# The last product of each expert group over 128 rows instead of 64, and at least one block per expert

## The chip, the cores and the metric

The kernel runs on one core of a Trainium2 chip. The metric is the time of one execution on the device in microseconds (us); lower is better.

## The reference, cut to what matters

Three stages follow each other. The first is a recurrent attention over 768 steps for 4 x 8 heads of 40. Its output, 3072 tokens of 320 numbers, goes through two mixtures of 8 experts with a hidden size of 1024:

```
# stage one: every token goes to one expert, at most 384 tokens each
logits = x @ w_gate
for idx in argsort(-logits.flatten()):          # best pairs first
    tok, e = idx // E, idx % E
    if assigned[tok] < 0 and counts[e] < cap:
        assigned[tok] = e; counts[e] += 1
out[mask] = maximum(x[mask] @ w1[e], 0) @ w2[e]

# stage two: every token goes to its best expert, without a limit
logits = (x / |x|) @ (emb / |emb|).T / tau
expert_idx = argmax(logits); gate_w = softmax(logits)[expert_idx]
for e in range(E):
    mask = expert_idx == e
    if not mask.any(): continue
    out[mask] = gate_w[mask] * (maximum(x[mask] @ w1[e], 0) @ w2[e])
```

The tokens of an expert in stage two are as many as fall to it: 324, 391, 241, 410, 350, 615, 235 and 506 for the inputs that the reference draws.

## The kernel before

Every engine has its own program, and semaphores order them. The attention takes the first 205 us or so, the routing of stage one goes on to about 450 us. The prediction is about the two expert stages behind it.

Float32 products are made of parts: a number is its high part (type fp32r) and a low part, what the rounding to the high part leaves. A product of w and x is w_hi x_hi + w_hi x_lo + w_lo x_hi, three matmuls. The 320 numbers of a token are three slices of the contraction, of 128, 128 and 64. For the third slice, w1_hi holds the high part of w1 in its rows 0 to 63 and the low part in rows 64 to 127, and xT_hi holds the same 64 numbers twice, so that one matmul over 128 rows (L1331, L1424) makes w_hi x_hi + w_lo x_hi. What is left is w_hi x_lo of the third slice, a matmul over the 64 rows 0 to LOW - 1 (L1332, L1425). It is the last of the eight that fill a PSUM bank, and carries the semaphore.

**Stage one** (step3, eight steps, one per expert, 384 tokens each). up3 goes through the eight 128-column parts f of the hidden layer: eight matmuls of 384 columns into bank f % 2. ACT takes the bank with a relu into hT_hi (L446), DVE makes hT_lo from bank and hT_hi (L959) and so frees the bank; PE waits for that before it fills the bank again, two parts later (hl3_done). Then turn3 transposes the tokens of the next expert (L1316), ACT and DVE make xT_hi and xT_lo of it (L439, L953), and down3 multiplies the hidden layer with w2 for three blocks of 128 tokens (L1304 to L1306). Between them lie the routing of stage two for the results of the step before: transposes (L1251), logits (L1361) and ranks (L1370).

**Stage two** (experts2, 31 blocks of 128 tokens, whose expert is read from a table). A step is: up(i), for two halves of the hidden layer, eight matmuls of 512 columns each; turn(i + 1), three transposes (L1407); down(i - 1); turn_hidden(i), eight transposes (L1443). ACT makes hid (L499), xT_hi (L503) and hT_hi (L514), DVE xT_lo (L1060), hT_lo (L1067) and the weighted result (L1072).

**The table** of stage two's blocks is computed by DVE after the last routing (L1108 to L1134): nblk is the number of blocks of each expert, cumb their running sum, and from it come the expert, the place of the weights and the first row of each block. row_ready (L1126) releases ACT's loads of token rows, tab_ready (L1134) the other engines. Of the 31 blocks those behind the last expert's are filling.

**The weights** of both stages pass through two places (RING). SP loads the raw w1 and w2 of an expert into one buffer each; it asks for w1 when POOL is done with the last w1, for w2 when POOL is done with the last w2. POOL copies raw weights by DMA into the high parts (L625, L627 for w1, L646 for w2), then subtracts to get the low parts (L634, L636, L652). In stage two SP also hands PE's progress on to POOL, behind its own loads in its queue:

```
done = sp.value_load(cumb_i[0:1, m:m + 1], min_val=0, max_val=NB2)
sp.wait_ge(h_ready, 2 * done + 1)
sp.sem_inc(slot1_free, 1)
sp.wait_ge(yb_ready, done + 1 + G)
sp.sem_inc(slot2_free, 1)
```

When POOL is done with the weights of the last expert, it scatters the results of stage two to the output, block by block (L682).

Of the kernel before, what the change touches and what calls it, by code (L numbers as in the profile page):

```python
# [45 lines left out]
KT = 3  # L46
# [20 lines left out]
class Chain:  # L67
# [14 lines left out]
    def link(self, ins):  # L82
        self.need(self.mark(ins))


def build(nc, t, out):
    ctx = ExitStack()
    with ctx:
# [598 lines left out]
        def _(dve):  # L687
# [261 lines left out]
            def x_lo3(e, p):  # L949

                for k in range(KT):
                    dve.wait_ge(xh3_ready, KT * e + k + 1)
                    V.tensor_tensor(xT_lo[:, k, :], bank[2 + k][:, 0:BPE * 128], xT_hi[:, k, :], ALU.subtract).then_inc(xl3_done, 1)  # L953
                V.tensor_copy(ids3[:, p, :], rows[:, :, XROW - 2]).then_inc(ids3_ready, 1)  # L954

            def hidden_lo3(e):
# [100 lines left out]
            def x_lo(i, s):  # L1057

                dve.wait_ge(xh_ready, i + 1)
                V.tensor_tensor(xT_lo[:, :, 0:128], bank[2][:, 0:384].rearrange("p (k t) -> p k t", k=KT), xT_hi[:, :, 0:128], ALU.subtract)  # L1060
                V.tensor_copy(ids[:, ds(i, 1)], rows[:, s, XROW - 2:XROW - 1])
                V.tensor_copy(weight[:, ds(i, 1)], rows[:, s, XROW - 1:XROW]).then_inc(x_done, 1)

# [28 lines left out]

            link(V.tensor_tensor(emb_sq[:, :], emb[:, :], emb[:, :], ALU.mult))
            V.tensor_reduce(emb_n[:, 0:1], emb_sq[:, :], AX.X, ALU.add).then_inc(sqrt_in, 1)
            V.memset(prev3[:, :, :], 0.0)
            V.tensor_copy(offset[:, :], region[:, :])
            link(V.reciprocal(tau[:, :], tau[:, :]))
# [12 lines left out]

            link(V.tensor_tensor(work[:, :, :], by_expert(rem[:, :]), g128[:, :, :], ALU.is_gt))
            link(V.tensor_reduce(nblk[:, :], work[:, :, :], AX.X, ALU.add))
            link(V.memset(full[:, :], 1.0))
            link(V.tensor_tensor_scan(cumb[:, :], full[:, :], nblk[:, :], 0.0, ALU.mult, ALU.add))

# [23 lines left out]
        def _(pe):  # L1139
# [179 lines left out]
            def up3(e, s):  # L1319

                pe.wait_ge(w1_ready, 2 * e + 2)
                pe.wait_ge(xl3_done, KT * (e + 2))
                for f in range(FT):
                    dst, cols = bank[f % 2][:, 0:BPE * 128], slice(f * 128, (f + 1) * 128)
                    pe.wait_ge(hl3_done, FT * e + f + 1)
                    for k in range(2):
                        T.matmul(dst, w1_hi[:, s, k, cols], xT_hi[:, k, :], start=(k == 0), stop=False)  # L1327
                        T.matmul(dst, w1_hi[:, s, k, cols], xT_lo[:, k, :], start=False, stop=False)  # L1328
                        T.matmul(dst, w1_lo[:, s, k, cols], xT_hi[:, k, :], start=False, stop=False)  # L1329

                    T.matmul(dst, w1_hi[:, s, 2, cols], xT_hi[:, 2, :], start=False, stop=False)  # L1331
                    T.matmul(dst, w1_hi[0:LOW, s, 2, cols], xT_lo[0:LOW, 2, :], start=False, stop=True).then_inc(h3_ready, 1)  # L1332

            def down3(e, s, b):
                dst, cols = bank[5 + b][:, 0:DM], slice(b * 128, (b + 1) * 128)
# [74 lines left out]
            def up(i):  # L1410
# [8 lines left out]
                for f in range(2):  # L1419
                    for k in range(2):  # L1420
                        products(bank[f][:, :], xT_hi[:, k, 0:128], xT_lo[:, k, 0:128],
                                 w1_part(w1_hi, 128, k, f), w1_part(w1_lo, 128, k, f), k == 0, False)

                    T.matmul(bank[f][:, :], xT_hi[:, 2, 0:128], w1_part(w1_hi, 128, 2, f), start=False, stop=False)  # L1424
                    T.matmul(bank[f][:, :], xT_lo[0:LOW, 2, 0:128], w1_part(w1_hi, LOW, 2, f), start=False, stop=True).then_inc(h_ready, 1)  # L1425

            def down(i):
                slot = pe.value_load(tab2[0:1, 0, ds(i, 1)], min_val=0, max_val=RING - 1)
# [106 lines left out]
```

## Time and profile before

| | us |
|---|---|
| median of 3 runs | 1084.75 |
| lowest, highest | 1078.61, 1091.55 |
| span of the profiled execution | 1103.3 |
| time of the profiled execution | not given beside its span |
| PE busy | 816.0 (74%) |
| DVE busy | 567.8 (51%) |
| POOL busy | 392.8 (36%) |
| ACT busy | 217.4 (20%) |

The span goes from the first to the last instruction of the execution that the profiler recorded; it is longer than any of the three runs. Busy shares are means over stages with different limits. PE stands for TensorE's matmuls and PEld for its weight loads, which have a row of their own; the ends of matmuls are modelled by the profiler, their starts are measured. A time that stands ahead of "<-" is idle time of the engine just before the instruction, and the name behind it is what ended it; "issue" means that nothing in the profile did.

### The profile page before, as it was taken

How to read it: one execution, taken by the hardware profiler on the slowest of the kernel's cores; microseconds unless marked ns; L12 is line 12 of the kernel's file. 1: busy time of each engine (PE TensorE's matmuls, PEld its weight loads, DVE VectorE, ACT ScalarE, POOL GpSimd, SP SyncE). 2: the span in 40 equal slices, each digit the busy share in tenths (PEclk: the TensorE clock that was granted, in tenths of full speed). 3: DMA queues.
4: the chain of work that ended last, by engine and by line, in shares of the span. 5: the costliest groups of instructions: out<-in, count | busy, mean ns of one | idle time of the engine just before them, and what ended most of it. 6: DMA issues, size and time to landing. Idle time of an engine off the chain costs nothing.

```text
span 1103.3 us, 18868 instructions
## 1 busy us (share of the span) xinstructions
PE 816.0 (74%) x5803; PEld 679.3 (62%) x5804; DVE 567.8 (51%) x1558; ACT 217.4 (20%) x451; POOL 392.8 (36%) x334
## 2 busy tenths in 40 slices
PE   2989888982233333039999999994799999998496
PEld 1777777861222222028888888874577888776385
DVE  7877778357766677302656566648222222222121
ACT  3221222000000000002332322331222222221121
POOL 4443334035200000533554465546034254356411
PEclk9998899695555555559999888996899999999699
DMA  4444443264300000233766576555454755653200
GB/s 133 136 142 119 130 119 107 68 196 127 122 0 0 0 0 0 78 109 83 247 193 189 185 236 197 150 175 172 132 174 125 215 171 167 191 156 118 89 27 1
DMA packets 70227, 137.26 MB, mean 124 GB/s; under 512 B 14791, under 2 KB 53968, under 8 KB 66098
## 3 DMA queue, kind: packets, MB, share of 16 engines
q1 hardware_dynamic: 43282, 67.16, 20.8%
q0 software_dynamic: 11008, 58.16, 16.2%
q10 hardware_dynamic: 15904, 11.53, 4.0%
q8 instruction: 17, 0.28, 0.1%
q14 instruction: 16, 0.13, 0.0%
HBM read 77.36 MB, written 14.48 MB: 83 GB/s over the span
## 4 chain that ended last, share of the span: by engine, by line
PE 53%; DVE 17%; issue 9%; another core or an unknown queue 1%; ACT 1%; DVEq 0%; POOL 0%; ACTq 0%; POOLq 0%
PE bank L1304 8%; PE bank L1305 7%; PE bank L1306 7%; PE bank L1290 4%; PE bank L1327 3%; PE bank L1425 2%; PE bank L1443 2%; PE bank L1332 2%; PE bank L1328 2%; PE bank L1329 2%; PE bank L1259 2%; PE bank L1361 2%; DVE routing_arena L859 2%; DVE routing_arena L892 2%; DVE routing_arena L954 1%
## 5 line engine op out<-in xcount | busy, mean ns | idle before, releaser
L1304 PE MATMUL bank<-w_hi,hT_hi 128*128 (+1 forms) x440 | 148.3, 337 | 19.1 <-issue 16.5
L1306 PE MATMUL bank<-w_hi,hT_lo 128*128 (+1 forms) x440 | 142.7, 324 | 1.8 <-issue 1.8
L1305 PE MATMUL bank<-w_lo,hT_hi 128*128 (+1 forms) x440 | 143.3, 326 | 1.0 <-issue 1.0
L1290 PE MATMUL bank<-routing_arena 128*8 128x16 bf16 x1344 | 43.3, 173 | 103.7 <-DVE routing_arena L859 103.7
L652 POOL TENSOR_TENSOR w_lo<-w_raw,w_hi 128x2560 fp32r<-128x2560 f32 x16 | 91.0, 5685 | 76.1 <-DMA w_hi<-w_raw 75.6
L606 POOL DMA_INDIRECT x_sorted<-tokens,routing_arena x48 | 47.3, 986 | 187.7 <-DVE routing_arena L942 161.6
L1290 PEld LDWEIGHTS bank<-routing_arena 128*8 128x8 bf16 x1344 | 37.5, 93 | 108.8 <-DVE routing_arena L859 108.8
L1304 PEld LDWEIGHTS bank<-w_hi,hT_hi 128*128 128x128 f32 x440 | 89.5, 203 | 21.9 <-issue 21.7
L634 POOL TENSOR_TENSOR w_lo<-w_raw,w_hi 128x2048 fp32r<-128x2048 f32 x16 | 73.0, 4564 | 69.0 <-DMA w_hi<-w_raw 68.1
L1305 PEld LDWEIGHTS bank<-w_lo,hT_hi 128*128 128x128 f32 x440 | 89.5, 203 | 1.8 <-issue 1.8
L1306 PEld LDWEIGHTS bank<-w_hi,hT_lo 128*128 128x128 f32 x440 | 89.1, 202 | 1.4 <-issue 1.4
L1060 DVE TENSOR_TENSOR xT_lo<-bank,xT_hi 128x384 fp32r<-128x384 f32 x31 | 17.3, 557 | 135.5 <-ACT xT_hi L503 135.5
L959 DVE SCALAR_TENSOR_TENSOR hT_lo<-bank,hT_hi 128x384 fp32r<-128x384 f32 x64 | 35.7, 557 | 80.2 <-ACT hT_hi L446 79.0
L625 POOL DMA_DIRECT2D w_hi<-w_raw x16 | 9.3, 582 | 160.5 <-PE bank L1332 79.7
L1202 PE MATMUL bank<-mlstm_arena 128*128 128x41 f32 (+3 forms) x384 | 62.1, 291 | 0.0
L1178 PE MATMUL bank<-mlstm_arena 128*128 128x256 f32 x192 | 55.6, 432 | 7.8 <-DVE mlstm_arena L736 7.8
L1304 PE MATMUL bank<-w_hi,xT_hi 128*128 x124 | 55.5, 447 | 7.4 <-issue 4.6
L1072 DVE TENSOR_SCALAR tokens<-bank,routing_arena 128x320 f32 (+1 forms) x31 | 17.1, 551 | 83.2 <-PE bank L1306 75.4
L725 DVE TENSOR_TENSOR_SCAN mlstm_arena<-bank,mlstm_arena 128x384 f32<-128x384 f32 x64 | 57.3, 940 | 3.7 <-PE bank L1167 3.2
L499 ACT ACTIVATE routing_arena<-bank 128x512 f32<-128x512 f32 x62 | 37.0, 600 | 112.3 <-PE bank L1425 94.7
L1202 PEld LDWEIGHTS bank<-mlstm_arena 128*128 128x128 f32 x384 | 57.8, 214 | 1.2 <-issue 0.2
L514 ACT ACTIVATE hT_hi<-bank 128x512 fp32r<-128x512 f32 x62 | 33.9, 596 | 118.7 <-PE bank L1443 98.8
(250 smaller groups left out, 1806.7 us busy)
## 6 DMA issues: line engine op xcount, KB each, us to landing
w_raw<-in_moe_w SPq DMA_DIRECT2D x16, 1280.0 KB, 6.7
w_hi<-w_raw POOLq DMA_DIRECT2D x16, 1280.0 KB
w_raw<-in_moe_w SPq DMA_DIRECT2D x16, 1024.0 KB
w_hi<-w_raw POOLq DMA_DIRECT2D x16, 1024.0 KB, 4.7
w_hi<-w_raw POOLq DMA_DIRECT2D x32, 256.0 KB, 5.8
mlstm_arena<-in_q SPq DMA_DIRECT2D x64, 120.0 KB
routing_arena<-x_sorted ACTq DMA_DIRECT2D x31, 160.0 KB
w_raw<-in_moe_w SPq DMA_DIRECT2D x16, 256.0 KB
```

Source lines behind the costliest of these rows:

```text
L499: nc.scalar.activation(hid[:, f * 512:(f + 1) * 512], bank[f][:, :], ACT.Relu).then_inc(relu_done, 1)
L606: pool.indirect_dma_start(dst, bass.IndirectOffsetOnAxis(ap=dest[:, g:g + 1], axis=0), tokens[:, slot, :], None).then_inc(scattered, 16)
L634: nc.gpsimd.tensor_tensor(w1_lo[:, s, :, :], w1_raw[:, 0:2, :], w1_hi[:, s, 0:2, :], ALU.subtract).then_inc(w1_ready, 1)
L652: nc.gpsimd.tensor_tensor(w2_lo[:, s, :, :], w2_raw[:, :, :], w2_hi[:, s, :, :], ALU.subtract).then_inc(w2_ready, 1)
L725: V.tensor_tensor_scan(decay[:, h, c], bank[f][:, 0:HALF], diag[:, :], 0.0, ALU.mult, ALU.add).then_inc(decay_done, 1)
L959: V.scalar_tensor_tensor(hT_lo[:, f, :], bank[f % 2][:, 0:BPE * 128], 0.0, hT_hi[:, f, :], ALU.max, ALU.subtract).then_inc(hl3_done, 1)
L1178: last = T.matmul(bank[2 + (NQ * k + g) % 2][:, c * QC:(c + 1) * QC], kT[:, s, chunk * CH:(chunk + 1) * CH], q_apart[:, s, chunk, :, :].re ...
L1202: last = T.matmul(bank[6 + s][:, at:at + n], probs[:, 2 * s + h, c * CH:(c + 1) * CH], v_in[:, 2 * s + h, c * DV:c * DV + n], start=(c == ...
L1290: last = T.matmul(bank[6][0:E, 0:WAYS], choice[:, :, g], cmp_b[:, g, :], start=(g == 0), stop=(g == G - 1))
L1304: T.matmul(dst, a_hi, b_hi, start=first, stop=False)
L1305: T.matmul(dst, a_hi, b_lo, start=False, stop=False)
L1306: return T.matmul(dst, a_lo, b_hi, start=False, stop=last)
```

## The change

- The matmuls L1332 and L1425, w1_hi by xT_lo of the third slice, take all 128 rows. Rows 64 to 127 of w1_hi hold w1's low part there.
- Rows 64 to 127 of xT_lo's third slice are cleared once (a memset of DVE ahead of stage one), so that they add nothing, and the instructions that write xT_lo leave them alone: in stage one the one for the third slice is cut to 64 partitions, in stage two one instruction for three slices becomes two (128 partitions by two slices, 64 by one).
- In the table of stage two the number of blocks of an expert is at least 1: one DVE instruction more.

```diff
@@ x_lo3 (DVE, stage one)
-                    V.tensor_tensor(xT_lo[:, k, :], bank[2 + k][:, 0:BPE * 128], xT_hi[:, k, :], ALU.subtract).then_inc(xl3_done, 1)
+                    V.tensor_tensor(xT_lo[0:KP[k], k, :], bank[2 + k][0:KP[k], 0:BPE * 128], xT_hi[0:KP[k], k, :], ALU.subtract).then_inc(xl3_done, 1)
@@ x_lo (DVE, stage two)
-                V.tensor_tensor(xT_lo[:, :, 0:128], bank[2][:, 0:384].rearrange("p (k t) -> p k t", k=KT), xT_hi[:, :, 0:128], ALU.subtract)
+                V.tensor_tensor(xT_lo[:, 0:2, 0:128], bank[2][:, 0:256].rearrange("p (k t) -> p k t", k=2), xT_hi[:, 0:2, 0:128], ALU.subtract)
+                V.tensor_tensor(xT_lo[0:LOW, 2, 0:128], bank[2][0:LOW, 256:384], xT_hi[0:LOW, 2, 0:128], ALU.subtract)
@@ DVE, ahead of stage one
+            V.memset(xT_lo[LOW:128, 2, :].bitcast(fp32), 0.0)
@@ DVE, table of stage two
             link(V.tensor_reduce(nblk[:, :], work[:, :, :], AX.X, ALU.add))
+            link(V.tensor_scalar(nblk[:, :], nblk[:, :], 1.0, None, ALU.max))
@@ up3 (PE, stage one)
-                    T.matmul(dst, w1_hi[0:LOW, s, 2, cols], xT_lo[0:LOW, 2, :], start=False, stop=True).then_inc(h3_ready, 1)
+                    T.matmul(dst, w1_hi[:, s, 2, cols], xT_lo[:, 2, :], start=False, stop=True).then_inc(h3_ready, 1)
@@ up (PE, stage two)
-                    T.matmul(bank[f][:, :], xT_lo[0:LOW, 2, 0:128], w1_part(w1_hi, LOW, 2, f), start=False, stop=True).then_inc(h_ready, 1)
+                    T.matmul(bank[f][:, :], xT_lo[:, 2, 0:128], w1_part(w1_hi, 128, 2, f), start=False, stop=True).then_inc(h_ready, 1)
```

## Rows read from the trace of the kernel before

**Rows 1.** The page, part 4: the chain that ended last, shares by engine.
```profile
PE 53%; DVE 17%; issue 9%; another core or an unknown queue 1%; ACT 1%; DVEq 0%; POOL 0%; ACTq 0%; POOLq 0%
```

**Rows 2.** Windows of 20 us: window, length, busy by engine, clock, DMA, GB/s.
```profile
core 0: us, PE busy (x) PEld busy (x) DVE busy (x) ACT busy (x) POOL busy (x), PEclk, DMA share, GB/s
...
640.00:660.00 20.00, 19.33 (x96) 17.08 (x96) 11.28 (x39) 6.65 (x14) 11.14 (x7) 0.83 0.80 251
...
880.00:900.00 20.00, 20.00 (x115) 16.53 (x114) 6.20 (x14) 6.43 (x12) 8.73 (x4) 1.00 0.52 156
...
1020.00:1040.00 20.00, 4.74 (x17) 4.20 (x18) 1.39 (x2) 1.45 (x3) 12.43 (x13) 0.59 0.31 111
```

**Rows 3.** Timeline of stage one, one group of eight products: start, length, engine, line.
```profile
655.33 0.44 PE L1332 MATMUL bank<-xT_lo,w_hi 64*128 64x384 f32 x1
...
655.80 0.49 ACT L446 ACTIVATE hT_hi<-bank 128x384 fp32r<-128x384 f32 x1 [1.23 <-PE bank L1332]
655.98 0.34 PE L1328 MATMUL bank<-xT_lo,w_hi 128*128 128x384 f32 x1
...
656.33 0.56 DVE L959 SCALAR_TENSOR_TENSOR hT_lo<-bank,hT_hi 128x384 fp32r<-128x384 f32 x1 [1.17 <-ACT hT_hi L446]
...
656.84 0.34 PE L1331 MATMUL bank<-xT_hi,w_hi 128*128 128x384 f32 x1
657.11 0.44 PE L1332 MATMUL bank<-xT_lo,w_hi 64*128 64x384 f32 x1
```

**Rows 4.** Timeline of stage two, across the end of a half in up.
```profile
986.22 0.39 PE L1424 MATMUL bank<-w_hi,xT_hi 128*128 x1
...
986.53 0.18 PEld L1425 LDWEIGHTS bank<-w_hi,xT_lo 64*128 64x128 f32 x1 [0.35 <-issue]
...
986.97 0.50 PE L1304 MATMUL bank<-w_hi,xT_hi 128*128 x1
...
987.30 0.39 PE L1305 MATMUL bank<-w_lo,xT_hi 128*128 x1
...
987.52 0.39 PE L1306 MATMUL bank<-w_hi,xT_lo 128*128 x1
```

**Rows 5.** Groups of weight loads by form, both stages: busy, mean ns, idle before.
```profile
L1332 PEld LDWEIGHTS bank<-xT_lo,w_hi 64*128 64x128 f32 x64 | 11.8, 184 | 16.2 <-issue 16.2
...
L1425 PEld LDWEIGHTS bank<-w_hi,xT_lo 64*128 64x128 f32 x62 | 11.3, 183 | 22.5 <-issue 22.5
```

**Rows 6.** Timeline of POOL in stage two: weights of experts 3, 4 and 7.
```profile
838.54 0.57 POOL L625 DMA_DIRECT2D w_hi<-w_raw  x1 [6.77 <-SPq L391]
...
845.42 4.59 POOL L634 TENSOR_TENSOR w_lo<-w_raw,w_hi 128x2048 fp32r<-128x2048 f32 x1 [5.28 <-DMA w_hi<-w_raw]
...
871.78 0.57 POOL L625 DMA_DIRECT2D w_hi<-w_raw  x1 [2.06 <-SPq L391]
...
882.09 4.59 POOL L634 TENSOR_TENSOR w_lo<-w_raw,w_hi 128x2048 fp32r<-128x2048 f32 x1 [8.71 <-DMA w_hi<-w_raw]
...
990.89 2.42 POOL L636 TENSOR_TENSOR w_hi<-w_raw,w_hi 64x1024 fp32r<-64x1024 f32 x1
```

**Rows 7.** Timeline of PE and ACT, 993 to 1042 us: block 23 and the hole.
```profile
993.87 0.47 PE L1304 MATMUL bank<-w_hi,xT_hi 128*128 x1
...
1002.24 1.03 PE L1443 MATMUL bank<-ident,routing_arena 128*128 128x128 f32 x8
...
1011.39 1.03 PE L1443 MATMUL bank<-ident,routing_arena 128*128 128x128 f32 x8
...
1022.77 0.60 ACT L514 ACTIVATE hT_hi<-bank 128x512 fp32r<-128x512 f32 x1 [14.19 <-remote]
...
1041.94 1.91 PE L1443 MATMUL bank<-ident,routing_arena 128*128 128x128 f32 x8
```

**Rows 8.** The page, part 5: DVE's subtraction of the tokens in stage two.
```profile
L1060 DVE TENSOR_TENSOR xT_lo<-bank,xT_hi 128x384 fp32r<-128x384 f32 x31 | 17.3, 557 | 135.5 <-ACT xT_hi L503 135.5
```

**Rows 9.** Timeline of DVE in the table of stage two.
```profile
766.57 0.16 DVE L1127 TENSOR_SCALAR routing_arena<-routing_arena 128x31 f32<-128x31 f32 x1
...
766.76 5.47 DVE L1128 TENSOR_SCALAR routing_arena<-routing_arena 128x31 f32<-128x31 f32 x1
```

## The prediction

> **What bounds the kernel now.** I read the chain that ended last first: over half of it is TensorE, with VectorE far behind [rows 1]. The windows then say where: in both expert stages (about 487 to 761 us and 775 us to the end) PE is busy for the whole of a window such as 880 to 900 us, at the full 2.4 GHz, while DVE, ACT and POOL are idle most of it [rows 2]. So there PE's own instructions set the time, and the question is how densely they follow each other. Two things interrupt this: in stage one part of each step runs at 1.2 GHz (window 640 to 660 has 0.83 of full speed, and 2 x 0.17 x 20 makes 6.8 us at half) [rows 2], and near the end, in window 1020 to 1040, there is a hole [rows 2], to which I return.
>
> Then the timeline of one group of eight products in stage one [rows 3]. Products with 128 rows start 0.172 us apart (655.98 to 656.84 is five of them). The product with 64 rows (L1332) starts 0.27 us after its forerunner (656.84 to 657.11), and from one L1332 to the next it is 1.78 us, where eight products at 0.172 make 1.38. In stage two [rows 4] the full products are 0.22 to 0.23 apart. The weight load of the 64-row product starts at 986.53, 0.31 after the matmul before it started and 0.08 before that one's end. The next matmul starts 0.43 after L1425's load, and the one behind it 0.33 later. A weight load of the same shape as its neighbour starts with the matmul ahead of it, so it is hidden; at each change of the row count it isn't. The grouped rows show that this is regular: 64 and 62 such loads, each preceded by an idle loader, 16.2 and 22.5 us in all, while a load itself takes the usual 0.18 us [rows 5].
>
> **Part one, 128 rows instead of 64, stage one (L1332, 64 times).** If the full-row product behaves like its seven neighbours, a group takes 1.38 instead of 1.78: 0.40 saved. What is late next is the eviction. From the start of L1332 it is 0.47 to ACT's start, 0.53 more to DVE's, and 0.56 for DVE [rows 3]; a full-row matmul ends about 0.1 earlier, so 1.46, and I estimate 0.04 to 0.1 for the way back to PE (ACT and DVE start 0.03 to 0.04 after the end of what they wait for). The bank is wanted again one product and one group after the start of L1332: 0.17 + 1.38 = 1.55. The two are equal within my reading. If PE has to wait, it also pays an unhidden load, 0.10 by the last step of [rows 4], every second group or every group, and the gain is near 0.32. I take 0.36, the middle. The last of the eight groups of a step leads into the down product, which waits for that same eviction in series, so I count 0.15 there. A step gains 7 x 0.36 + 0.15 = 2.7, eight steps 21 us (18 to 25).
>
> **Part one, stage two (L1425, 62 times).** For the first half of the hidden columns, 986.22 to 987.30 is 1.08 where three pitches of 0.23 are 0.69: 0.39. The second half is followed by small transposes, which hide the last 0.10: 0.29. A block gains 0.68, and 31 blocks would give 21 us. I don't count all of it, since weights are supplied by POOL at a pace of its own. POOL's copy for expert 3 began at 838.54, released by the SP line that passes on PE's progress; for expert 4 at 871.78, where it had only just finished the work before (idle 2.06) [rows 6]. From there the supply is a closed loop (SP issues the next raw load when POOL is done, POOL waits for DMA), and PE's progress doesn't enter. The third slice of the last expert's w1 was ready at 990.89 + 2.42 = 993.31, and PE's block 23, the first of that expert, started at 993.87 [rows 6, 7]: a margin of 0.6 us. With 0.68 less per block PE would be there 23 x 0.68 = 15.6 us earlier, and finds no weights.
>
> How far does the supply itself come forward? Its last release by PE is the one at 838.54, after the seventh block: 7 x 0.68 = 4.8 us earlier. But then POOL's copy meets the raw load of w2 that SP has just issued. For expert 3 the wait for this copy was 5.28, for expert 4, where it met that load, 8.71 [rows 6], a difference of 3.4; moving into part of that load costs an estimated 1.8 of the 4.8. So the supply moves by 3 us (1.4 to 4.8) and block 23 with it. After it 7 blocks of 0.68 are PE's own: 4.8. Stage two gains 3 + 4.8 = 7.8. PE's new waits, 15.6 - 3 = 12.6 us shared by the later experts, may let the clock fall, as it does in the hole below (window 1020 to 1040 at 0.59) [rows 2]; I give 0 to 3 us for this and take 0, since what a slower clock costs ahead of the next wait is taken off that wait.
>
> **The hole.** From PE's turn of the hidden rows at 1002.24 to the next at 1011.39 is 9.15; to the one after it 30.55, so 21.4 us are lost [rows 7]. ACT stood still for 14.19, by a release that the profile can't name, although its input was there; POOL meanwhile issues its saved-up output scatters back to back (13 POOL instructions in window 1020 to 1040) [rows 2]. They start when POOL's last weights are done, wherever PE is, and both move by about 3 us here, so I keep the loss as it is, with 8 us either way.
>
> **Part two, the rest.** The subtraction of stage two (L1060, 557 ns, 31 times) becomes two instructions; one more costs DVE at most another 0.56 per block, during the down product, and DVE waited 135.5 us in all before it, more than 4 per block [rows 8]: nothing. Should that cover go, it is 0.56 per block. The clearing of xT_lo's lower rows runs once while all engines wait for the scatters before stage one: nothing. In stage one the subtraction only has fewer partitions. The bound of at least one block per expert adds one small DVE instruction ahead of the block table, about 0.2 us, the distance from L1127 to L1128. There DVE is about to be held: L1128, 31 elements a row like L1127, took 5.47 us in place of 0.16 [rows 9]. One instruction more means that a different one is held, with up to two left for later: 0 to 0.6 us; I take 0.2. It changes no block count if every expert has tokens, and the release of POOL at 838.54 just after seven blocks fits the counts of the reference's own inputs (3, 7, 9, 13, 16, 21, 23, 27 blocks cumulated), where the least is two.
>
> **A rule against this change.** What the rows show is that a 64-row load lasts 0.18 us like the full ones [rows 5], and only the waiting differs. The Trainium skill (TensorE: Matmul & The Clock Gate, Part 2, on LDWEIGHTS) says that the row count doesn't matter for the load's time; taken alone that gives a gain of nothing. The Trainium skill (TensorEngine Tiling (Array Packing), Key Properties) says "Changing tiling mode (not just tile) drains the TensorE", which is what the two gaps look like; by it the whole of both gaps goes. Rows here have the gaps but not their cause.
>
> **The sum.** 21 + 7.8 - 0.2 = 28.6, say 29 us. The profiled execution spans 1103.3 us and would span 1074; no other time of it is given. It lies 18.6 above the median of the runs, 1084.75, part of which may be the hole. Carried over as it is: 1084.75 - 29 = 1056.
>
> **Rivals.** (a) The weights don't hold stage two (POOL's loop shortens too): 21 + 21, stage one at up to 25: 1039 to 1043. Against it: POOL's waits are DMA times. 10%. (b) The gaps aren't due to the rows but to the last product of a group (its semaphore, its operand), so the change doesn't do what it says: 1085. For it: every 64-row product is also the last of its accumulation, so the rows can't separate them. Against: the loader is idle ahead of the 64-row load too [rows 5], and no semaphore stands between L1424 and L1425 in the code. 8%. The rule of the Trainium skill (TensorE: Matmul & The Clock Gate, Part 2) that the row count doesn't matter ends here too. (c) Slower: the clock. Stage one spends some 6.8 us of a step at 1.2 GHz [rows 2]; each us there costs 0.5. If the new waits (on evictions in stage one, on weights in stage two) keep PE at 1.2 GHz for 58 us more, the 29 are used up, at 100 more it is 1084.75 + 21 = 1106. Against: in stage one the waits are hundredths of a us, and full-row products raise the load. 3%. (d) The forecast's mechanism with the hole grown or shrunk: inside the range.
>
> **Chances.** Forecast 79%, (a) 10%, (b) 8%, (c) 3%. The range: low end (a), 1039. High end: stage one 18, stage two 5, the hole 8 longer, gives 1070, and 4 for a median of three runs that spread over 13: 1074. One per cent, 10.8 us, is about what a measurement of this kernel can tell from nothing. Faster by over 1%: 0.87 (forecast nearly whole, (a)); within: 0.10; slower: 0.03.
>
> **What the profile after would show.** The idle time ahead of the loads of L1332 and L1425 gone, groups of 1.38 to 1.46 us in stage one, the step shorter by 2.5 to 3 us; blocks of 8.5 us in stage two, and new PE waits of 4 us or so ahead of an expert's first block, above all block 23, released by POOL's L636; the table's DVE instructions held as before; the hole in the same place. I'd be wrong if the gap stays ahead of the last product, if PE doesn't wait before block 23, or if the hole changes by over 8 us.

## The result, and the profile after

| | before | changed |
|---|---|---|
| median, us | 1081.68 (4 runs) | 1053.20 (4 runs) |
| lowest, highest | 1078.25, 1091.55 | 1047.95, 1055.98 |
| span of the profiled execution | 1103.3 | 1051.0 |
| its time | - | 1052.89 |

The ratio is 0.9718, with a 95% interval of 0.9669 to 0.9767: 28.5 us between the medians and 30.5 between the means, from which the ratio is taken (25 to 36 by its interval), where 29 were forecast. The median of before was 1084.75 over three runs in the prediction; with the fourth it is 1081.68, so the forecast of 1056 lies 2.8 above the measured 1053.20. The time is 1.9 above the span (1052.89 and 1051.0).

The page of the changed kernel, part 1 and the shares of the chain that ended last (part 4), which answer to [rows 1]:

```profile
PE 768.7 (73%) x5803; PEld 683.1 (65%) x5804; DVE 572.6 (54%) x1591; ACT 216.4 (21%) x451; POOL 392.9 (37%) x334
...
PE 38%; DVE 18%; issue 10%; DMA 8%; POOL 6%; ACT 1%; SPq 0%; DVEq 0%; ACTq 0%; POOLq 0%
```

PE's share of the chain fell from 53% to 38%, and DMA and POOL now hold 14%: from block 23 the chain goes back through the supply of weights. PE lost 47 us of busy time (816.0 to 768.7), since the gaps had counted as busy. Against a second profile of before, which has no hole (e1, below), it is 43.5 us (812.2 to 768.7) for a span that is 30.0 shorter (1081.0 to 1051.0): some 13.5 us of what the full-row products saved came back as idle time of PE, 4 in stage one and 10 in stage two.

**Stage one.** The changed kernel's timeline of PE, PEld, ACT and DVE, where L1330 to L1334 are the seven full products and L1335 is the last one, now over 128 rows. It answers to [rows 3]:

```profile
643.36 0.34 PE L1335 MATMUL bank<-xT_lo,w_hi 128*128 128x384 f32 x1
...
644.27 0.56 DVE L959 SCALAR_TENSOR_TENSOR hT_lo<-bank,hT_hi 128x384 fp32r<-128x384 f32 x1 [0.95 <-ACT hT_hi L446]
...
644.61 0.33 PE L1334 MATMUL bank<-xT_hi,w_hi 128*128 128x384 f32 x1
...
644.78 0.34 PE L1335 MATMUL bank<-xT_lo,w_hi 128*128 128x384 f32 x1
644.88 0.19 PEld L1330 LDWEIGHTS bank<-xT_hi,w_hi 128*128 128x128 f32 x1
644.96 0.36 PE L1330 MATMUL bank<-xT_hi,w_hi 128*128 128x384 f32 x1
```

L1335 follows its forerunner by 0.17 (644.61 to 644.78) where it was 0.27, and a group takes 1.42 (643.36 to 644.78) where it took 1.78. The load at 644.88 doesn't start with L1335, as loads do elsewhere in the group, but 0.10 later and 0.05 after the end of DVE's eviction (644.27 + 0.56): that is the new limit. The groups by form, which answer to [rows 5], show no idle time before the last product in stage one and 2.6 us in all in stage two, where there were 22.5:

```profile
L1335 PEld LDWEIGHTS bank<-xT_lo,w_hi 128*128 128x128 f32 x64 | 12.2, 191 | 0.0
...
L1428 PEld LDWEIGHTS bank<-w_hi,xT_lo 128*128 128x128 f32 x62 | 11.9, 192 | 2.6
```

From the first transpose of stage one to the first of stage two (the eight steps and the table) it is 269.49 us (483.69 to 753.18). Before it was 288.44 in the profile that the prediction used, 285.71 in a second one (below). That is 16 to 19 us.

**Stage two.** The timeline of PE across the end of the first half, which answers to [rows 4]:

```profile
889.92 0.39 PE L1427 MATMUL bank<-w_hi,xT_hi 128*128 x1
890.15 0.39 PE L1428 MATMUL bank<-w_hi,xT_lo 128*128 x1
890.38 0.39 PE L1307 MATMUL bank<-w_hi,xT_hi 128*128 x1
```

All are 0.23 apart. A block without a wait takes 8.38 instead of 9.16, so 0.78 less where 0.68 was forecast. From 753.18 to the end it is 297.82 us; before it was 327.99, or 305.7 without the hole (21.4, and 0.9 in the block behind it, whose turn of the hidden rows comes after 10.04 instead of 9.15), and 307.85 in the second profile. That is 8 to 10 us of the 24 that 31 blocks of 0.78 would make. Where the rest went is seen at POOL and PE, whose timelines answer to [rows 6, 7]:

```profile
813.23 0.57 POOL L625 DMA_DIRECT2D w_hi<-w_raw  x1 [6.38 <-SPq L391]
...
964.59 2.34 POOL L636 TENSOR_TENSOR w_hi<-w_raw,w_hi 64x1024 fp32r<-64x1024 f32 x1
```

```profile
967.17 0.79 PE L1307 MATMUL bank<-w_hi,xT_hi 128*128 x1 [3.28 <-POOL w_hi L636]
967.76 0.63 PE L1308 MATMUL bank<-w_lo,xT_hi 128*128 x1
...
973.21 0.39 PE L1427 MATMUL bank<-w_hi,xT_hi 128*128 x1
```

PE waits for the weights of the last expert (block 23) by name, 3.28 us. Then its products last 0.63 instead of 0.39 for 6 us: 1.2 GHz (the granted clock of the window 967 to 973 is 0.50). One other wait for weights is named, 2.25 us for L652 at 913.01, behind the first block of the sixth expert. Besides waits for DVE of 4.6 us, which were there before, the rest of PE's idle time in stage two has no name in the trace: "issue" ahead of blocks, up to 1.45 us at once, 8 us in all, where the second profile of before has 4. Counted from stage two's start, the release for expert 3 is at 60.05 (before 63.23), the end of the last third slice at 213.75 (before 218.0), and block 23 at 213.99 (before 218.56).

**The hole** is not there. POOL's burst of scatters runs from 979.02, and the blocks beside it take 8.37.

### The profile page after: what moved, and what is told of

The parts are those of the page before. It is cut to its first block, busy times and chain, and to the rows that moved or that the text cites. A ratio compares the mean times of both kernels' runs of the same rounds, so it can differ in the third digit from the quotient of the medians.

```text
span 1051.0 us, 18901 instructions
## 1 busy us (share of the span) xinstructions
PE 768.7 (73%) x5803; PEld 683.1 (65%) x5804; DVE 572.6 (54%) x1591; ACT 216.4 (21%) x451; POOL 392.9 (37%) x334
## 3 DMA queue, kind: packets, MB, share of 16 engines
q1 hardware_dynamic: 43282, 67.16, 21.4%
## 4 chain that ended last, share of the span: by engine, by line
PE 38%; DVE 18%; issue 10%; DMA 8%; POOL 6%; ACT 1%; SPq 0%; DVEq 0%; ACTq 0%; POOLq 0%
DMA w_hi<-w_raw 8%; PE bank L1307 5%; PE bank L1308 4%; PE bank L1309 4%; PE bank L1293 4%; PE bank L1330 2%; PE bank L1262 2%; POOL w_lo L634 2%; PE bank L1331 2%; PE bank L1332 2%; POOL w_lo L652 2%; PE bank L1364 2%; DVE routing_arena L859 2%; DVE routing_arena L892 2%; DVE routing_arena L954 2%
## 5 line engine op out<-in xcount | busy, mean ns | idle before, releaser
L1308 PE MATMUL bank<-w_lo,hT_hi 128*128 (+1 forms) x440 | 141.0, 320 | 0.0
L652 POOL TENSOR_TENSOR w_lo<-w_raw,w_hi 128x2560 fp32r<-128x2560 f32 x16 | 91.1, 5692 | 72.9 <-DMA w_hi<-w_raw 72.4
L634 POOL TENSOR_TENSOR w_lo<-w_raw,w_hi 128x2048 fp32r<-128x2048 f32 x16 | 73.0, 4564 | 72.3 <-DMA w_hi<-w_raw 71.5
L1060 DVE TENSOR_TENSOR xT_lo<-bank,xT_hi 128x256 fp32r<-128x256 f32 x31 | 13.2, 425 | 119.0 <-ACT xT_hi L503 119.0
L959 DVE SCALAR_TENSOR_TENSOR hT_lo<-bank,hT_hi 128x384 fp32r<-128x384 f32 x64 | 35.7, 558 | 58.3 <-ACT hT_hi L446 58.3
L1307 PE MATMUL bank<-w_hi,xT_hi 128*128 x124 | 53.3, 430 | 13.1 <-issue 7.0
L1205 PE MATMUL bank<-mlstm_arena 128*128 128x41 f32 (+3 forms) x384 | 59.8, 283 | 0.2 <-ACT mlstm_arena L429 0.2
L1205 PEld LDWEIGHTS bank<-mlstm_arena 128*128 128x128 f32 x384 | 55.4, 205 | 1.6 <-issue 0.5
```

What stands on the lines that cost most here:

```text
L634: nc.gpsimd.tensor_tensor(w1_lo[:, s, :, :], w1_raw[:, 0:2, :], w1_hi[:, s, 0:2, :], ALU.subtract).then_inc(w1_ready, 1)
L652: nc.gpsimd.tensor_tensor(w2_lo[:, s, :, :], w2_raw[:, :, :], w2_hi[:, s, :, :], ALU.subtract).then_inc(w2_ready, 1)
L959: V.scalar_tensor_tensor(hT_lo[:, f, :], bank[f % 2][:, 0:BPE * 128], 0.0, hT_hi[:, f, :], ALU.max, ALU.subtract).then_inc(hl3_done, 1)
L1205: last = T.matmul(bank[6 + s][:, at:at + n], probs[:, 2 * s + h, c * CH:(c + 1) * CH], v_in[:, 2 * s + h, c * DV:c * DV + n], start=(c == ...
L1307: T.matmul(dst, a_hi, b_hi, start=first, stop=False)
L1308: T.matmul(dst, a_hi, b_lo, start=False, stop=False)
```

## The experiments

Ratios are to the kernel before in runs on the same chip in the same job. Medians of before were 1082.61 (e1 to e4), 1082.76 (e5 to e8) and 1106.85 (e9 to e12); in the third job every kernel profiled had the hole, so absolute times are compared within a job only.

**e1_before_again.** The kernel before, unchanged, with a profile.

> The kernel before, profiled once more. My theory takes the hole near the end (21.4 us between two turns of the hidden rows while POOL issues its saved-up scatters, and all engines stand) for an accident of the one profiled execution, since the profile of the changed kernel has the same burst of scatters and no hole: here it is absent or of another size, the span is 1076 to 1090 us, and stage two takes some 306 us instead of 328. Rival, that the hole belongs to the kernel before and the change removed it: it is there again with 20 us or more, and the span is about 1103.

Time 1082.86, span 1081.0, stage two 307.85. The timeline of PE across block 23 and later:

```profile
1000.55 1.03 PE L1443 MATMUL bank<-ident,routing_arena 128*128 128x128 f32 x8
...
1009.70 1.04 PE L1443 MATMUL bank<-ident,routing_arena 128*128 128x128 f32 x8
...
1018.92 1.03 PE L1443 MATMUL bank<-ident,routing_arena 128*128 128x128 f32 x8
```

The turns are 9.15 and 9.22 apart, where [rows 7] have 30.55. The hole belonged to that execution, not to the kernel, and it made up the distance to the median: the profiled time would be 1103.3 + 1.9, 20.5 above 1084.75, for a hole of 21.4 (22.3 with the slower block behind it).

**e2_stage1_only** and **e3_stage2_only.** Before, with part one in one stage alone (the clearing and the cut subtraction come with either).

```diff
  e2: up3
-  T.matmul(dst, w1_hi[0:LOW, s, 2, cols], xT_lo[0:LOW, 2, :], start=False, stop=True).then_inc(h3_ready, 1)
+  T.matmul(dst, w1_hi[:, s, 2, cols], xT_lo[:, 2, :], start=False, stop=True).then_inc(h3_ready, 1)
  e3: up
-  T.matmul(bank[f][:, :], xT_lo[0:LOW, 2, 0:128], w1_part(w1_hi, LOW, 2, f), start=False, stop=True).then_inc(h_ready, 1)
+  T.matmul(bank[f][:, :], xT_lo[:, 2, 0:128], w1_part(w1_hi, 128, 2, f), start=False, stop=True).then_inc(h_ready, 1)
```

> Part one in stage one alone; stage two keeps its 64-row products. Theory (each change of the row count costs 0.2 us of TensorE's time, twice a group): 19 to 21 us less than before, ratio 0.981, groups of 1.42 us instead of 1.79, stage two as before. Rival, that the last product of a group waits for another reason: in this kernel also gone, so it doesn't tell those apart; rival that the gain came from stage two or from chance: ratio over 0.99.

> Part one in stage two alone. Theory: blocks of 8.38 instead of 9.16 us where PE is free, but PE then waits for POOL's weights, so that of 31 x 0.78 = 24 us only 8 to 10 come out: ratio 0.991 to 0.993. Rival (the supply doesn't bind): 22 to 24 us, ratio 0.979.

e2: 0.9855 (0.9824 to 0.9887), stage one 268.34, stage two 307.73, unchanged. e3: 0.9929 (0.9896 to 0.9962), stage one 286.02, stage two 297.72. So the parts have their gains where they are made, 15.7 and 7.7 us, and one doesn't feed the other; their sum of 23.4 is below the 30.5 that the ratio of the whole change makes, and agrees with it just within the intervals (3.4, 3.6 and 5.3 us). e2 stays below its forecast; the step that lacks is told below.

**e4_rows64_middle.** The rival that the gap belongs to the last product and not to its rows: the 64-row product is moved into the middle of the group, and a 128-row product is last and carries the semaphore. (The same in up.)

```diff
                         T.matmul(dst, w1_lo[:, s, k, cols], xT_hi[:, k, :], start=False, stop=False)
+                        if k == 0:
+                            T.matmul(dst, w1_hi[0:LOW, s, 2, cols], xT_lo[0:LOW, 2, :], start=False, stop=False)
-                    T.matmul(dst, w1_hi[:, s, 2, cols], xT_hi[:, 2, :], start=False, stop=False)
-                    T.matmul(dst, w1_hi[0:LOW, s, 2, cols], xT_lo[0:LOW, 2, :], start=False, stop=True).then_inc(h3_ready, 1)
+                    T.matmul(dst, w1_hi[:, s, 2, cols], xT_hi[:, 2, :], start=False, stop=True).then_inc(h3_ready, 1)
```

> The kernel before with the 64-row product moved from the last place of each group of eight to the fourth, in both stages; the last is now the 128-row product of the third slice. Theory (the cost lies at the change of the row count): the two gaps move with it, group 1.78 us, block 9.16 us, ratio 0.997 to 1.003. Rival (it is the last product with its semaphore that waits): no gap ahead of the fourth product, one stays at the end or none at all; if none, the ratio is near 0.972.

1.0034 (0.9995 to 1.0072). Timeline of PE and PEld, stage one; L1331 is the 64-row product, L1333 the last:

```profile
654.94 0.34 PE L1329 MATMUL bank<-xT_hi,w_lo 128*128 128x384 f32 x1
655.21 0.18 PEld L1331 LDWEIGHTS bank<-xT_lo,w_hi 64*128 64x128 f32 x1 [0.25 <-issue]
655.21 0.44 PE L1331 MATMUL bank<-xT_lo,w_hi 64*128 64x384 f32 x1
...
655.58 0.19 PEld L1327 LDWEIGHTS bank<-xT_hi,w_hi 128*128 128x128 f32 x1 [0.19 <-issue]
...
656.21 0.33 PE L1333 MATMUL bank<-xT_hi,w_hi 128*128 128x384 f32 x1
...
656.38 0.33 PE L1327 MATMUL bank<-xT_hi,w_hi 128*128 128x384 f32 x1
```

The idle time of the loader went with the 64-row product, on both of its sides (0.25 and 0.19), while the last product of the group is followed at 0.17. A block of stage two without a wait takes 9.20 to 9.21 (before 9.15 to 9.16). Rival (b) is refuted.

**e5_rows64_pairs.** If the cost lies in the change of the row count, two 64-row products side by side should pay it once: the product is last in every even group and first in every odd one.

```diff
+                    if f % 2:
+                        T.matmul(dst, w1_hi[0:LOW, s, 2, cols], xT_lo[0:LOW, 2, :], start=True, stop=False)
...
-                    T.matmul(dst, w1_hi[0:LOW, s, 2, cols], xT_lo[0:LOW, 2, :], start=False, stop=True).then_inc(h3_ready, 1)
+                    if f % 2 == 0:
+                        last = T.matmul(dst, w1_hi[0:LOW, s, 2, cols], xT_lo[0:LOW, 2, :], start=False, stop=True)
+                    last.then_inc(h3_ready, 1)
```

> The kernel before with the 64-row product last in even groups and first in odd ones, so that two of them stand side by side: two changes of the row count per two groups instead of four, with as many 64-row products. Theory (the cost is the change): two groups take 2 x 1.38 + 0.40 = 3.16 us or a little more for the eviction, where 2 x 1.79 stood; stage one gains about half of the 19, stage two blocks of 8.77, held by the weights in part; 13 to 17 us, ratio 0.984 to 0.988. Rival (each 64-row product costs 0.4 wherever it stands): ratio 1.000.

0.9908 (0.9874 to 0.9943). Timeline of PE and PEld, the two side by side (L1335, L1327) and the next pair:

```profile
656.45 0.34 PE L1333 MATMUL bank<-xT_hi,w_hi 128*128 128x384 f32 x1
...
656.72 0.44 PE L1335 MATMUL bank<-xT_lo,w_hi 64*128 64x384 f32 x1
656.82 0.19 PEld L1327 LDWEIGHTS bank<-xT_lo,w_hi 64*128 64x128 f32 x1
657.00 0.34 PE L1327 MATMUL bank<-xT_lo,w_hi 64*128 64x384 f32 x1
...
657.26 0.19 PEld L1329 LDWEIGHTS bank<-xT_hi,w_hi 128*128 128x128 f32 x1 [0.25 <-issue]
...
659.91 0.44 PE L1335 MATMUL bank<-xT_lo,w_hi 64*128 64x384 f32 x1
```

Two groups take 3.19 (656.72 to 659.91), where they took 2 x 1.78: one of the two costs of 0.40 is gone. The second 64-row load has no idle time before it. A block takes 8.80, halfway to 8.38. The total gained 10 us (0.9908 of 1082.76), less than the 13 to 17 expected: in stage one the third step took 35.43, of which more below, and stage two was held by the weights (the interval of block 23 is 15.8). The Trainium skill (TensorEngine Tiling (Array Packing), Key Properties) has it that a change of the tiling mode drains TensorE; e4 and e5 agree, at 0.40 us for a change of the row count and the change back; what TensorE does in that time no run shows.

**e6_short_lows.** Is it the supply of the weights that holds stage two? For the experts of stage two that POOL fills during the stage, the subtractions for w1_lo and w2_lo cover 64 of 1024 and 16 of 320 columns; the other low parts stay those of an earlier expert. This leaves out part of the computation.

```diff
-  nc.gpsimd.tensor_tensor(w1_lo[:, s, :, :], w1_raw[:, 0:2, :], w1_hi[:, s, 0:2, :], ALU.subtract).then_inc(w1_ready, 1)
+  nf = F if n < E + RING else 64
+  nc.gpsimd.tensor_tensor(w1_lo[:, s, :, 0:nf], w1_raw[:, 0:2, 0:nf], w1_hi[:, s, 0:2, 0:nf], ALU.subtract).then_inc(w1_ready, 1)
```

> The changed kernel, where POOL computes only 64 of the 1024 columns of w1's low part and 16 of the 320 of w2's for experts 2 to 7 of stage two; the rest of the low parts is that of older weights. Theory (PE waits for POOL's weights in stage two): POOL's loop shortens by some 9 us an expert, PE's waits ahead of experts and the slow clock behind the longest go, 12 to 16 us less than the changed kernel, ratio 0.957 to 0.961. Rival (the waits have another source, such as fetching instructions or the loads themselves): the waits stay, ratio 0.97.

0.9637 (0.9571 to 0.9703); stage two 288.37, 9.4 less than with the change alone, and no PE wait on POOL is left. So by the profiles weights held some 9 of the missing 14 to 16 us. The 12 to 16 expected were not reached, and in time the kernel is only 0.8% below the change alone (0.9718), with intervals that overlap. What remains are seven idle times of PE of 0.9 to 1.8 us that the trace gives to nothing; e1 has four of 0.8 to 1.0, so they aren't new.

**e7_early_copies.** The whole computation, with the supply loop changed: SP passes PE's progress on before it asks for the next raw load, and POOL issues w1's copy ahead of the subtraction for w2, so that the copy runs beside it.

The part on POOL (SP's lines are only moved):

```diff
-                split_weights(n)
+                load_hi1(n)
+                if n > E + RING:
+                    make_lo2(n - 1)
+                make_lo1(n)
+                load_hi2(n)
+            make_lo2(2 * E - 1)
```

> The changed kernel with the full computation; SP passes PE's progress on ahead of the raw load of w2, and POOL issues the copy of an expert's w1 before it subtracts for the last expert's w2, and the copy of w2 without waiting for its landing, as in stage one. Theory: the DMA waits of POOL (some 20 us of a loop of 34) lie beside its subtractions, PE doesn't wait in stage two: 12 to 16 us less than the changed kernel, ratio 0.957 to 0.961. Rival (the DMA queues are the bound, so the copies land no earlier when more of them overlap): under 4 us, ratio 0.968 to 0.972.

0.9687 (0.9613 to 0.976); stage two 290.78, 7.0 less than with the change alone. POOL's timeline shows the loop turned round:

```profile
871.72 0.55 POOL L624 DMA_DIRECT2D w_hi<-w_raw  x1 [12.57 <-SPq L367]
...
873.35 5.68 POOL L651 TENSOR_TENSOR w_lo<-w_raw,w_hi 128x2560 fp32r<-128x2560 f32 x1
879.18 4.62 POOL L633 TENSOR_TENSOR w_lo<-w_raw,w_hi 128x2048 fp32r<-128x2048 f32 x1
```

POOL waits 12.57 for PE's progress instead of 8 to 10 for a DMA: the copy is hidden behind L651. No PE wait on POOL is left here either, with the whole computation, so e6's gain doesn't hang on the work that it leaves out. In the profile this is the best stage two of the full computation, though 7.0 is half of the 12 to 16 expected; in time it can't be told from the change alone (0.9718).

**e8_short_eviction.** Why 1.42 and not 1.38 in stage one: DVE's eviction (L959) writes 128 of 384 columns. The low part of the hidden layer is left out for the rest.

```diff
-  V.scalar_tensor_tensor(hT_lo[:, f, :], bank[f % 2][:, 0:BPE * 128], 0.0, hT_hi[:, f, :],
+  V.scalar_tensor_tensor(hT_lo[:, f, 0:128], bank[f % 2][:, 0:128], 0.0, hT_hi[:, f, 0:128],
```

> The changed kernel, where in stage one DVE computes hT_lo for 128 of the 384 tokens of each group (the rest is zero), so that the eviction of a group is some 0.27 us shorter. Theory (a group takes 1.42 us instead of 1.38 because PE waits for the eviction every second group): groups of 1.38, and the down product starts 0.27 sooner: 2.2 + 2 = 4 us, ratio 0.968. Rival (1.42 is what the products take): groups of 1.42 and 2 us for the down product alone.

0.9723 (0.9656 to 0.9791). The last products start at 645.41, 646.79 and 648.18, 1.38 apart, so the 0.04 was the eviction, as the prediction had it. Its value was not found: of 4 us expected the last steps gave 0.3 each (30.8 instead of 31.1), and stage one as a whole took 269.21, since its third step had grown to 35.49. A step loses more elsewhere, as e11 shows.

**e9_pe_four_blocks** and **e10_all_four_blocks.** The idle times of PE that e6 and e7 left could belong to the loop in PE's program (two blocks a turn). e9 is e7 with four blocks a turn on PE, e10 with ACT and DVE as well.

```diff
-                with pe.Fori(0, NB2 // 2 - 1) as j:
-                    step(2 * j + 1, lambda: turn(2 * j + 2, 0, j + 2))
-                    step(2 * j + 2, lambda: turn(2 * j + 3, 1, j + 2))
+                with pe.Fori(0, (NB2 // 2 - 1) // 2) as j:
+                    step(4 * j + 1, lambda: turn(4 * j + 2, 0, 2 * j + 2))
...
+                    step(4 * j + 4, lambda: turn(4 * j + 5, 1, 2 * j + 3))
```

> The kernel of e7 (earlier copies), with TensorE's loop over the blocks of stage two unrolled to four blocks a turn, seven turns in place of fourteen; the instructions of a block are the same. Theory: with the weights there, what is left between the blocks (idle 0.3 to 1.8 us that no semaphore ends, mostly ahead of an up at the loop's end, only while weights are copied) is the fetching of instructions behind the jump; with half the jumps half of it goes, 3 to 5 us less than e7, ratio 0.964 to 0.966. Rival (it comes with the transfers, wherever the loop ends): as e7, 0.9687.

> As e9, with the loops of ACT and DVE over the blocks unrolled to four as well. Theory: their jumps are off the path, so this is as e9 within 2 us. Rival (their fetching delays the blocks too): 2 us or more below e9.

e9: 0.9674 (0.9611 to 0.9738), e10: 0.9645 (0.958 to 0.971), e7 had 0.9687: no difference that can be told, though the intervals of 7 us either way leave room for the 3 to 5 us expected. The trace decides more: PE's timeline in e9, with half the jumps, still has the idle times:

```profile
880.13 0.49 PE L1311 MATMUL bank<-w_hi,xT_hi 128*128 x1 [1.37 <-issue]
```

Their cause stays open. Both profiles contain the hole (block intervals of 21.8 and 18.1 in e9), so it also comes in kernels with the change.

**e11_short_lows_stage1.** Where do stage one's steps lose time? The theory is that POOL's subtractions hold DVE. The cut of e6, but for the weights that are made during stage one (RING up to E + RING) in place of those of stage two; again part of the computation is left out.

```diff
+                nf = F if not RING <= n < E + RING else 64
...
+                nd = DM if not RING <= n < E + RING else 16
```

> The changed kernel, where POOL computes only 64 of 1024 columns of w1's low part and 16 of 320 of w2's for the weights that it prepares during stage one (those of experts 2 to 7 of stage one and the first two of stage two); the rest is older. Theory: small DVE instructions on SBUF are held while POOL subtracts (5.3 to 5.6 us for 128 x 3), and in the step whose third-to-last place this takes the path PE waits 3 us for the logits; with short subtractions no DVE instruction is held over 1 us, the step of 34.6 us falls to 31 and each other step loses its 0.7 to 0.9 us wait ahead of L1364: 6 to 10 us less than the changed kernel, ratio 0.963 to 0.967. Rival (the hold costs nothing but that one step): 3 us, ratio 0.969. Rival (the step is longer for its transfers): no change, 0.972.

0.951 (0.9447 to 0.9572): more than any theory said. Stage one takes 242.82 instead of 269.49, its later steps 27.2 instead of 31.1. The changed kernel first, timeline of POOL, DVE and PE in its fourth step:

```profile
561.06 5.70 POOL L652 TENSOR_TENSOR w_lo<-w_raw,w_hi 128x2560 fp32r<-128x2560 f32 x1
561.20 5.58 DVE L954 COPY routing_arena<-routing_arena 128x3 f32<-128x3 f32 x1
566.71 0.15 DVE L965 COPY tokens<-routing_arena 128x3 f32<-128x3 f32 x1
...
567.07 4.53 POOL L634 TENSOR_TENSOR w_lo<-w_raw,w_hi 128x2048 fp32r<-128x2048 f32 x1 [0.31 <-DMA w_hi<-w_raw]
567.17 0.40 DVE L984 COPY routing_arena<-bank 128x256 f32<-128x256 f32 x1
...
568.96 2.29 PE L1364 MATMUL bank<-gate_weights,routing_arena 128*128 128x8 f32 x13 [0.67 <-DVE routing_arena L985]
```

A copy of three elements a row begins 0.14 after POOL's subtraction, ends with it and takes 5.58; its like takes 0.15. DVE's copies for the logits come late by that, and PE waits 0.67. Then the windows of 2 us (length, busy by engine, clock, DMA, GB/s), the changed kernel:

```profile
568.00:570.00 2.00, 1.33 (x11) 1.03 (x9) 1.23 (x5) 1.92 (x7) 2.00 (x1) 1.00 0.88 206
570.00:572.00 2.00, 2.00 (x11) 1.93 (x11) 0.64 (x3) 1.97 (x3) 1.92 (x2) 0.58 1.05 387
572.00:574.00 2.00, 2.00 (x8) 1.98 (x9) 2.00 (x1) 0.56 (x1) 2.00 (x1) 0.50 1.04 331
574.00:576.00 2.00, 2.00 (x10) 2.00 (x9) 1.69 (x10) 0.00 (x0) 0.04 (x1) 0.50 0.40 62
576.00:578.00 2.00, 2.00 (x12) 2.00 (x11) 0.72 (x6) 0.22 (x1) 0.00 (x0) 0.72 1.03 422
```

and e11 at the same place of the step:

```profile
570.00:572.00 2.00, 2.00 (x16) 2.00 (x15) 1.07 (x5) 1.95 (x5) 0.00 (x0) 1.00 0.97 313
572.00:574.00 2.00, 2.00 (x16) 1.94 (x15) 1.09 (x2) 1.61 (x3) 1.56 (x2) 1.00 1.07 388
```

PE was busy 1.33 of 2.00, and then the clock is down for four windows: 2 x (0.42 + 0.50 + 0.50 + 0.28) makes 3.4 us lost. With the wait of 0.67 that is 4.1, about the 3.9 by which a step is shorter in e11, where PE has no gap here and stays at 2.4 GHz. But the sum mustn't be read as clock 3.4 and hold 0.5, since the changed kernel has a step in which the clock did not fall. The fifth, PE's timeline and the window between:

```profile
600.00 2.64 PE L1364 MATMUL bank<-gate_weights,routing_arena 128*128 128x8 f32 x18 [0.67 <-DVE routing_arena L985]
602.00:604.00 2.00, 2.00 (x15) 1.96 (x16) 1.51 (x3) 1.66 (x3) 1.92 (x2) 1.00 1.09 365
607.81 0.19 PE L1373 MATMUL bank<-routing_arena,tri 128*128 128x24 bf16 x1 [1.46 <-DVE routing_arena L1005]
```

The wait is the same 0.67 and the clock stays at 1.00, but the step still takes 29.87: PE, being earlier, waits another 1.46 for DVE at the ranks. So of the 3.9 us some 2.7 (29.87 to 27.2) are DVE's lateness, and 1.2 (31.1 to 29.87) is what the fall of the clock adds. Nor does a fall need a wait. In e11's third step, where PE's largest idle time is 0.27, the window is

```profile
547.00:549.00 2.00, 2.00 (x9) 2.00 (x8) 1.37 (x9) 0.22 (x1) 0.00 (x0) 0.50 0.92 358
```

after two windows with PE busy throughout. What decides whether the clock falls behind these small products isn't shown. The Trainium skill (SBUF — State Buffer, Who interferes with whom) says that GpSimd and a VectorE copy or scalar operation in a two-port mode share one pair of ports, which the first to come keeps for its whole instruction. The trace agrees in what can be timed: 5.58 for L954 beside L652, while L984, whose input is in PSUM, takes its 0.40 beside L634.

**e12_block_min_only.** Before, with part two alone.

```diff
+            link(V.tensor_scalar(nblk[:, :], nblk[:, :], 1.0, None, ALU.max))
```

> Part two alone: at least one block per expert, 64-row products as before. Every expert has tokens, so the blocks are the same; one small DVE instruction more, 0.2 us: ratio 0.998 to 1.002. Rival (it pushes an instruction that releases ACT's row loads into the hold by POOL's subtraction): 1 to 5 us slower, ratio 1.001 to 1.005.

0.9994 (0.9954 to 1.0035): nothing that can be measured; a cost of up to 3.8 us isn't excluded by the times. In its profile the hold falls on the same instruction as before.

## Why the prediction was right, step by step

The mechanism. That TensorE loses time at a product with fewer rows than its neighbours was read from two gaps; e4 shows that they go with the rows and e5 that they lie at the change of the row count. Rivals (b) and (c) didn't come; the gap is gone in both stages. That 28.6 and 28.5 agree to 0.1 is luck: stage one gave 2 to 5 us less than its term and stage two 0 to 2 more, the parts alone (e2, e3) sum to 23.4, and the measurement is good to 5 us.

**Stage one, 21 us (18 to 25): 16 to 19 measured.** The group was given as 1.42 (a gain of 0.36) between 1.38 and 1.46, and is 1.42; the eviction as what is late next is shown by e8. Steps 4 to 7 together are 10.5 (against e1) to 11.5 us shorter, 2.6 to 2.9 each, for 2.7 forecast. The term was mis-sized in one step: the third takes 34.60 where it took 33.18 (32.79 in e1). The timeline of the changed kernel there:

```profile
528.85 5.69 POOL L652 TENSOR_TENSOR w_lo<-w_raw,w_hi 128x2560 fp32r<-128x2560 f32 x1
529.24 5.33 DVE L965 COPY tokens<-routing_arena 128x3 f32<-128x3 f32 x1 [2.49 <-PE bank L1309]
...
536.68 1.01 PE L1364 MATMUL bank<-gate_weights,routing_arena 128*128 128x8 f32 x4 [2.98 <-DVE routing_arena L985]
```

POOL waits for a raw load there (its copy at 527.23 had waited 10.31), which moves less than PE: counted from stage one's start the subtraction comes 3.0 us earlier (45.16, before 48.21), DVE's copy 5.1 (45.55, before 50.69). So the copy falls almost wholly under the subtraction (5.33; before 3.25), PE waits 2.98 for the logits instead of 0.90, and the clock of the step is 0.85 instead of 0.95. The prediction asked of a faster PE what is late next within a group, but not what the step then meets in POOL's program. That is 4.1 us (2.7 forecast and not gained, and 1.4 lost). It is no accident of one run: over all profiles this step takes 33.8 to 35.5 in the kernels that have the change in stage one and POOL's subtractions whole, and 32.8 to 33.2 in the others with the 64-row product last.

**Stage two, 7.8 us: 8 to 10 measured.** Its structure was right: 24 us would be there for the taking, the weights hold most of what doesn't come, PE waits before block 23 for L636, and the supply itself moves only a little. In terms, from the profiles before and after: up to block 23 3 us was forecast and 4.6 measured (218.56 to 213.99). Both halves of that term were off and made up for each other: the release moved by 3.2, not 4.8, and the 1.8 taken off for the meeting with w2's raw load didn't come (the wait for this copy is 5.33, before 5.28; the last third slice moved by 4.3). Behind it 7 blocks x 0.68 = 4.8 was forecast; it is 8 blocks, 23 to 30, x 0.78 = 6.2, less 2.8 for the clock (from its first product to the next block's, 967.17 to 978.30, block 23 takes 11.13 instead of 8.38): 3.5, and 3.3 is measured without the hole. The clock was taken as 0 of 0 to 3, because its cost would be taken off the next wait; behind block 23 there is no next wait. The waits of 4 us or so ahead of an expert's first block, the sign that the prediction named, came at block 23 alone; the time that PE has too much before is spent in the idle times without a name, ahead of every second or third block. The 0.78 is 0.39 for each half, since the transposes behind the second half hid nothing of the gap.

Rival (a) didn't come in the changed kernel, but e6 shows what it stood on: with the supply shortened, stage two loses 9.4 more.

**The table, 0.2: right, and within nothing.** Before, L1128 was held 5.47; now it is L1131, which is the same instruction, one line pushed down by the new one and two by others:

```profile
741.64 0.17 DVE L1115 TENSOR_SCALAR routing_arena<-routing_arena 128x8 f32<-128x8 f32 x1
...
745.15 5.45 DVE L1131 TENSOR_SCALAR routing_arena<-routing_arena 128x31 f32<-128x31 f32 x1
```

It begins 0.15 after a POOL subtraction (745.00, 5.57) and ends with it, as L954 does at 561.20; that the hold would pass to another instruction was wrong, here and in e12.

**The hole.** The prediction kept it and carried the distance to the median over. The time came out right, but by the subtraction and not by the reading: the hole was in the profile and not in the median. By the prediction's own sign (a hole that changes by over 8 us) this part of it was wrong. The spans differ by 52.3 (1103.3 and 1051.0), and 22.3 of it is the hole; the remaining 30 are 19.0 of stage one, 7.9 of stage two and 3.2 ahead of stage one, where nothing was changed and where the other profiles of before and of the single parts scatter as much (482.6 to 490.5).

## What to carry to other kernels

In a dense stream of matmuls look at the start-to-start distance, not at the busy time: here a product over fewer rows than its neighbours cost more than a full one, and the zero rows cost nothing, since the operands already lay there. When PE gets faster, walk the other engines' programs once more for what does not move with it (a DMA loop of weights, an engine that holds another). Look at the granted clock behind each PE wait instead of assuming it, and before a slow stretch is charged to the clock, look for a step in which the clock didn't fall: the wait next in line may take most of it back. Before a feature of one profile goes into a sum, compare the profile's own time with the median of the runs: a hole that makes up the difference isn't in the median.

## What the runs showed of the hardware that was not expected

- A DVE instruction on three elements a row took 5.58 us beside a POOL subtraction of 5.70, in five of the eight steps of stage one, before and after. With those subtractions cut to a few columns a step took 27.2 instead of 31.1 us, the largest effect found here. A version of the full computation without the hold was not tried.
- The clock behind the small products of the logits differs from step to step in one execution. In the changed kernel the same wait of 0.67 us was followed by some 6.8 us at 1.2 GHz in three steps and by none in the fifth; in e11 the clock was at 0.50 in the third step without a wait. A wait of 3.28 us in stage two stood ahead of 6 us at 1.2 GHz.
- One 64-row product among 128-row ones costs 0.40 us in all with 384 columns and 0.39 with 512. Of two side by side the second starts 0.28 behind the first (656.72 to 657.00), not 0.17, although its load has no idle time before it.
- The hole (20 to 25 us near the end) was in the first profile of before and in all four of the third job, but in none of the eight of the first two; it comes with the job, not with the change, and the second and third job ran on the same chip. What it is stays open, as do the idle times of 1 to 1.8 us that PE has ahead of some blocks of stage two.
